# Reordering attention's tail, adding a second set of partial sums in the ELU stage, and loading the output weights in pieces

## The reference

```
kv  = einsum('bhsd,bhse->bhde', k, v)
o   = einsum('bhsd,bhde->bhse', q, kv)
x   = o / sqrt(mean(o*o, -1) + 1e-6) * g_norm      # -> [4608, 512]
x   = (sigmoid(x @ w_gate) * (x @ w_val)) @ w_out  # inner width 1536
h   = x @ w_in                                     # inner width 2048
out = where(h > 0, h, exp(min(h, 0)) - 1) @ w_out2 # [4608, 512]
```

## Time and profile before

| | us |
|---|---|
| median of 3 runs | 1703.28 (1703.05 to 1709.16) |
| profiled execution | 1700.83 |
| its span | 1698.7 |
| TensorE matmul busy | 1639.0 (96%) |
| DVE busy | 1198.8 (71%) |
| ACT busy | 819.1 (48%) |
| GpSimd busy | 181.7 (11%) |

### The profile page before, as it was taken

One profiled execution on the slowest core, in us unless ns is written; L12 is line 12 of the kernel. 1 busy time (PEld: TensorE's weight loads), 2 busy tenths in 40 slices (PEclk: granted clock), 3 DMA queues, 4 the chain that ended last, 5 costly groups with the idle time before them and its releaser, 6 DMA issues.

```text
span 1698.7 us, 27990 instructions
## 1 busy us (share of the span) xinstructions
PE 1639.0 (96%) x10920; PEld 1613.1 (95%) x10920; DVE 1198.8 (71%) x1429; ACT 819.1 (48%) x1251; POOL 181.7 (11%) x185
## 2 busy tenths in 40 slices
PE   6996999999999999999999999999999899999999
PEld 5776999999999999999999999999999799999999
DVE  5777888887588754777777666776765676766764
ACT  6664555554455443444444444554454444444443
POOL 6564222220022100000000000000000000000000
PEclk9998999999999999999999999999999999999999
DMA  9993488878788456554333754423329833333341
GB/s 279 283 293 130 161 309 314 311 292 318 257 302 313 175 180 228 206 226 142 137 137 140 284 193 140 149 105 138 139 103 347 300 128 125 125 124 125 133 145 55
DMA packets 194745, 339.35 MB, mean 200 GB/s; under 512 B 13376, under 2 KB 149568, under 8 KB 194624
## 3 DMA queue, kind: packets, MB, share of 16 engines
q1 hardware_dynamic: 194624, 337.69, 56.6%
HBM read 191.89 MB, written 145.75 MB: 199 GB/s over the span
## 4 chain that ended last, share of the span: by engine, by line
PE 75%; DVE 6%; ACT 4%; issue 4%; DMA 2%; SPq 1%; POOL 0%; ACTq 0%; DVEq 0%; POOLq 0%
PE pair L898 38%; PE pair L963 21%; PE pair L931 15%; DVE s L1393 3%; DVE e L1498 2%; ACT e L1187 1%; DMA u_elu<-s 1%; ACT s L1206 1%; ACT e L1223 1%; ACT e L1218 1%; DMA wreg<-weight_items 1%; DMA weight_items<-out_w 0%; ACT s L1197 0%; ACT ring L1083 0%; SPq L493 0%
## 5 line engine op out<-in xcount | busy, mean ns | idle before, releaser
L898 PE MATMUL pair<-ring,wreg 128*128 128x384 f32 x5040 | 887.7, 337 | 25.5 <-ACT s L1206 15.5
L898 PEld LDWEIGHTS pair<-ring,wreg 128*128 128x128 f32 x5040 | 879.7, 189 | 32.6 <-ACT s L1206 20.9
L963 PE MATMUL pair<-wreg,ring 128*128 128x256 f32 x3024 | 364.8, 284 | 6.6 <-DMA wreg<-weight_items 6.6
L963 PEld LDWEIGHTS pair<-wreg,ring 128*128 128x128 f32 x3024 | 364.6, 193 | 6.8 <-DMA wreg<-weight_items 6.8
L1393 DVE TENSOR_TENSOR s<-s,pair 128x768 f32<-128x768 f32 (+1 forms) x252 | 210.7, 836 | 179.4 <-PE pair L898 144.3
L931 PE MATMUL pair<-ring,wreg 128*128 128x384 f32 x1512 | 262.2, 334 | 0.0
L931 PEld LDWEIGHTS pair<-ring,wreg 128*128 128x128 f32 x1512 | 262.1, 188 | 0.0
L1317 DVE TENSOR_TENSOR ring<-raw,ring 128x1024 fp32r<-128x1024 f32 (+1 forms) x162 | 180.7, 1134 | 112.3 <-ACT ring L1093 97.3
L1187 ACT ACTIVATE e<-e 128x768 f32<-128x768 f32 x72 | 61.0, 847 | 185.9 <-DVE e L1498 185.9
L1093 ACT ACTIVATE ring<-raw 128x1024 fp32r<-128x1024 f32 x108 | 111.8, 1051 | 55.7 <-DVE raw L1351 41.3
L1317 DVE TENSOR_TENSOR ring<-sum,ring 128x768 fp32r<-128x768 f32 (+1 forms) x90 | 92.3, 1038 | 30.2 <-ACT ring L1093 13.5
(11 more groups left out here) (98 smaller groups left out, 1475.5 us busy)
## 6 DMA issues: line engine op xcount, KB each, us to landing
wreg<-weight_items SPq DMA_DIRECT2D x98, 512.0 KB, 6.8
raw<-u_elu SPq DMA_DIRECT2D x36, 1024.0 KB, 7.4
u_gated<-ub SPq DMA_DIRECT2D x144, 192.0 KB, 2.8
u_elu<-s SPq DMA_DIRECT2D x72, 384.0 KB, 2.4
weight_items<-out_w SPq DMA_DIRECT2D x50, 512.0 KB, 4.6
weight_items<-out_x SPq DMA_DIRECT2D x48, 512.0 KB, 4.7
x_raw<-x_attention SPq DMA_DIRECT2D x48, 384.0 KB, 5.2
raw_k<-u_gated SPq DMA_DIRECT2D x6, 2304.0 KB, 8.4
```

The lines of the kernel that those rows point to most:

```text
L898: mm = pe.matmul(dst[:, g, 0:NT], w[:, a, cols], ring[:, slot, b, kt, :], start=(i in STARTS and kt == a == b == 0), stop=(kt == 1 and a = ...
L963: mm = pe.matmul(dst[:, 0, 0:256], s[:, b, 2 * c + kt, :], w[:, a, cols], start=(i in STARTS and c == kt == a == b == 0), stop=(c == 3 and ...
```

## The change

- The small buffers of attention are laid out anew, so that rinv, r_hi and r_lo no longer lie under s1, s5 and s2. ACT copies P1 after step 33 and P6 after step 35, P5 first after attention. TensorE does P6 directly behind P2, and steps 35 and 36 after it.
- S3, S2, S1, S4 of the first superblock stand after steps 25, 26, 27, 28, the splits of P1 and P2 after steps 28 and 29, the others at 32 to 36. SP loads the superblock after step 24 instead of 28. GpSimd makes three of chunk 1's four sums after steps 25, 26 and 27.
- In the ELU stage even units use s1b, s5b, s2b, odd ones s1, s5, s2; copies wait for the store of two units before. P1's split of the next superblock moves from unit j = 3 (i = 0) to j = 2 (i = 6). raw4_1's first half is loaded in unit 65 instead of 64.
- Output weights: in each unit of the last visit SP loads the cells of that unit's own buffer after P2 (two cells), P7 (three) and P4 (two). In unit 65 the last two follow after the unit and after raw4_1's second half.

```diff
-                 ("sq", [P, 2, HN], F32, 69 * KIB),
...
+                 ("rinv", [P, HN], F32, 69 * KIB),
+                 ("r_hi", [P, 2, HN], F32R, 69 * KIB + 1152),
+                 ("r_lo", [P, 2, HN], F32R, 69 * KIB + 3456),
+                 ("sq", [P, 2, HN], F32, 69 * KIB + 5760),
+                 ("sq_hi", [P, 2, 2, HN], F32R, 69 * KIB + 8064),
+                 ("sq_lo", [P, 2, 2, HN], F32R, 69 * KIB + 12672),
...
+                ("s1b", [P, 2, NT], F32, 69 * KIB),
+                ("s5b", [P, 2, NT], F32, 72 * KIB),
+                ("s2b", [P, 2, NT], F32, 75 * KIB),
...
+        def parts3(n):
+            return {"11": s1b, "12": s2b, "22": s5b} if n % 2 == 0 else {"11": s1, "12": s2, "22": s5}
...
@@ SP @@
-                if p == PAIRS - NP:
+                if p == PAIRS - RING:
...
-                    if j > 0 and at == 0 and last:
-                        sp.wait_ge(s_prod, prod(n - 1, P4))
-                    if j == 2 and at == 0 and last:
+                    if n == FIRST4 - 1 and at == 2:
+                        for m in range(4):
+                            sp.wait_ge(s_st[m], 16 * n)
                         load_raw4(1, (0,))
...
-                    if last and j > 0:
-                        load_out_cells(BUF3[j - 1], pieces)
+                    if last and at > 0:
+                        items = ((0, 1), (2, 3, 4), (5, 6))[at - 1]
+                        if n < FIRST4 - 1:
+                            sp.wait_ge(s_prod, prod(n, items[-1]))
+                            load_out_cells(BUF3[j], items)
+                        elif at < 3:
+                            sp.wait_ge(s_prod, prod(n, items[-1]))
+                            load_out_cells(BUF3[j], items)
                     store_elu(n, c)
             sp.wait_ge(s_prod, prod(FIRST4 - 1, P4))
-            load_out_cells(BUF3[3], range(4))
             for c in range(2):
                 sp.wait_ge(s_st[c], 16 * FIRST4)
             load_raw4(1, (1,))
-            load_out_cells(BUF3[3], range(4, 7))
+            load_out_cells(BUF3[3], (5, 6))
@@ GpSimd @@
-            static_steps(step, PAIRS - RING, PAIRS + LM + 1)
-            for c in range(1, CHUNKS):
+            static_steps(step, PAIRS - RING, PAIRS - RING + 2)
+            weight_sums(1, (0,))
...
+            static_steps(step, PAIRS - RING + 4, PAIRS + LM + 1)
+            weight_sums(1, (3,))
+            for c in range(2, CHUNKS):
                 weight_sums(c)
@@ TensorE @@
             gated_product(0, P2)
-            static_steps(step, PAIRS + 3, PAIRS + 4)
             gated_product(0, P6)
-            static_steps(step, PAIRS + 4, PAIRS + 5)
+            static_steps(step, PAIRS + 3, PAIRS + 5)
@@ ACT @@
+            def first_unit():
+
+                copy_p5(0)
+                fill1(0, 0)
+                fill1(0, 1)
+                sigmoid(0, "11")
...
@@ in fill3, ACT and DVE @@
-                elif j == UNITS3 - 1 and vis + 1 < NS:
+                elif j == UNITS3 - 2 and vis + 1 < NS and i == 6:
+                    split_x2(vis + 1, P1)
+                elif j == UNITS3 - 1 and vis + 1 < NS and i > 0:
                     split_x2(vis + 1, i)
@@ elu_unit, ACT; the same for "12" and "22" @@
-                act.wait_ge(s_st[0], 16 * n)
+                act.wait_ge(s_st[0], 16 * (n - 1))
                 if n == FIRST3:
                     act.wait_ge(s_sum, summed(2, NS - 1, "S4"))
-                act.activation(s1[:, :, :], pa[:, :, 0:NT], ACT.Copy).then_inc(s_snap, 1)
+                    act.wait_ge(s_lo, split2(NS - 1, P4, 2))
+                act.activation(part["11"][:, :, :], pa[:, :, 0:NT], ACT.Copy).then_inc(s_snap, 1)
@@ end of attention, ACT @@
+                if p == PAIRS + 1:
+                    act.wait_ge(s_ms, PAIRS)
+                    copy_p1(0)
+                if p == PAIRS + 3:
+                    copy_p6(0)
+                for i in {PAIRS - 4: (P1,), PAIRS - 3: (P2,), PAIRS: (P6,), PAIRS + 1: (P5,), PAIRS + 2: (P7,),
+                          PAIRS + 3: (P3,), PAIRS + 4: (P4,)}.get(p, ()):
                     split_x1(0, i)
-            act.wait_ge(s_ms, PAIRS)
-            act.wait_ge(s_rlo, B)
-            for n in range(FIRST2):
+            first_unit()
+            for n in range(1, FIRST2):
                 gated_unit(n)
@@ DVE @@
+            def first_unit():
+
+                combine(0, "11", s1[:, :, :], PC[:, :, 0:NT])
+                combine(0, "22", s5[:, :, :], PA[0][:, :, 0:NT])
+                fill1(0, 0)
+                fill1(0, 1)
+                gate(0, "11")
...
-                for name in {PAIRS - 2: ("S3", "S2"), PAIRS + 1: ("S1",), PAIRS + 2: ("S4",)}.get(p, ()):
-                    sum_x(1, 0, name)
+                if PAIRS - 7 <= p < PAIRS - 3:
+                    sum_x(1, 0, SUMS[p - (PAIRS - 7)])
```

More of the change, by code:

```diff
@@ L766, in _, with weight_sums @@
             pool.wait_ge(s_const, CONSTANTS)
-            def weight_sums(c):
+            def weight_sums(c, parts=range(4)):
                 t1, t2 = (by_item(staging(c)[1][:, n, :], c) for n in range(2))
                 b11, b12, b21, b22 = (quarter(c, kh, fh) for kh in range(2) for fh in range(2))
[L772 to L778, removed]
-                pool.wait_ge(s_wsum, 4 * c + 3)
-                pool.wait_ge(s_wlo, ITEMS * c + P2 + 1)
-                pool.tensor_tensor(b21, b21, t2, ALU.subtract).then_inc(s_wsum, 1)
+                if 0 in parts:
+                    if c >= 1:
+                        pool.wait_ge(s_wlo, ITEMS * (c - 1) + P5 + 1)
+                    pool.wait_ge(s_wraw[c % 2], raw_loaded(c))
+                    pool.tensor_tensor(t1, b12, b11, ALU.subtract).then_inc(s_wsum, 1)
+                if 1 in parts:
+                    pool.tensor_tensor(b12, b22, b12, ALU.subtract).then_inc(s_wsum, 1)
+                if 2 in parts:
+                    pool.wait_ge(s_wsum, 4 * c + 1)
+                    pool.tensor_tensor(t2, b22, t1, ALU.subtract).then_inc(s_wsum, 1)
+                if 3 in parts:
+                    pool.wait_ge(s_wsum, 4 * c + 3)
+                    pool.wait_ge(s_wlo, ITEMS * c + P2 + 1)
+                    pool.tensor_tensor(b21, b21, t2, ALU.subtract).then_inc(s_wsum, 1)
             def step(trip, r, valid):
@@ L1131, in gated_unit @@
                     act.wait_ge(*c21_taken(n - 1))
-                act.activation(sg[:, :], pa[:, 0, 0:NT], ACT.Sigmoid).then_inc(s_sig, 1)
+                act.activation(sg[:, :], PA[n % 2][:, 0, 0:NT], ACT.Sigmoid).then_inc(s_sig, 1)
+            def first_unit():
[3 more added lines that the diff above has]
+                sigmoid(0, "11")
+                fill1(0, 2)
+                sigmoid(0, "22")
+                fill1(0, 3)
+                fill1(0, 4)
+                sigmoid(0, "12")
+                fill1(0, 5)
+                fill1(0, 6)
+                sigmoid_c21(0)
+            def gated_unit(n):
+                fill1(n, 0)
+                copy_p1(n)
+                fill1(n, 1)
+                sigmoid(n, "11")
+                fill1(n, 2)
+                copy_p6(n)
+                fill1(n, 3)
+                copy_p5(n)
+                fill1(n, 4)
+                sigmoid(n, "22")
+                fill1(n, 5)
+                sigmoid(n, "12")
+                fill1(n, 6)
+                sigmoid_c21(n)
             def mid_unit(n):
@@ L1489, in elu_unit @@
                 e0, e1 = e_3
+                part = parts3(n)
                 def minimum(c, e, acc):
@@ L1505, in elu_unit @@
                 fill3(n, 0)
-                combine(n, "11", s1[:, :, :], PC[:, :, 0:NT])
-                minimum("11", e0, s1)
+                combine(n, "11", part["11"][:, :, :], PC[:, :, 0:NT])
+                minimum("11", e0, part["11"])
                 fill3(n, 1)
-                result(0, e0, s1)
+                result(0, e0, part["11"])
                 fill3(n, 2)
                 fill3(n, 3)
-                combine(n, "22", s5[:, :, :], pa[:, :, 0:NT])
-                minimum("22", e1, s5)
+                combine(n, "22", part["22"][:, :, :], pa[:, :, 0:NT])
+                minimum("22", e1, part["22"])
                 fill3(n, 4)
-                result(1, e1, s5)
-                combine(n, "12", s2[:, :, :], PB[:, :, 0:NT])
-                minimum("12", e0, s2)
+                result(1, e1, part["22"])
+                combine(n, "12", part["12"][:, :, :], PB[:, :, 0:NT])
+                minimum("12", e0, part["12"])
                 fill3(n, 5)
-                result(2, e0, s2)
+                result(2, e0, part["12"])
                 fill3(n, 6)
```

97 lines of the change are left out of this document (51 added, 46 removed).

## The result

The changed kernel takes 1696.39 us in the median of 8 runs (1691.59 to 1697.99), the kernel before 1703.4 (8 runs, 1702.91 to 1709.16). The ratio is 0.9947, 95% interval [0.9937, 0.9957]: so 7 us faster by the medians and 9 by the ratio, where I forecast 25. The direction was right, the size not; 1696.39 lies outside my range of 1667 to 1691. The profiled execution after took 1696.32 us (span 1694.2), the one before 1700.83.

What follows compares the result with a forecast made beforehand. TensorE was taken as the bound nearly everywhere, with time to win only at its gaps or halved clock. 12.8 + 6.3 - 0.8 + 6.8 = 25.1 us off 1703.28 gave about 1678, range 1667 to 1691.

Steps and rivals of the forecast that it cites:

- P1 to P7: Unit 0 at attention's end: replay from P1's start at 139.7 to P7's at 153.2, before the 4.5 us shift.
- The pipeline reaches step 30 4.5 us later.: Attention steps 25 to 29: sums and splits moved there, x_raw's landing and GpSimd delay step 30 by 4.5 us (bounds 1, 8).
- the uneven fit: Attention steps 25 to 29: six moved sums and splits fit DVE's idle time in total but not evenly; 1.5 us charged.
- Unit 1: "take 1.5.": Unit 1, after attention: DVE's backlog makes P4 come out 1 to 2 us late, taken as 1.5 us lost.
- Second set: 6.3 less, 0.8 against it.: ELU stage: removed store waits and about 1 us of clock gain 6.3 us; 0.8 us charged for e1's store.
- rival 4: Last visit, ELU stage: e1's store lands late and holds DVE's minimum; 2.8 us in each of four units, 11; chance 0.04.
- Output weights: 6.8.: Start of the output stage: loading in pieces leaves 1.5 of the 6.61 us gap and removes 1.7 us of half clock.
- attention and gated stage 12.8: Term A, attention's tail and first units: 11.6 + 2.7 - 1.5 = 12.8 us less (bounds 3 and 19).
- ELU 5.5: ELU stage: the second set's 6.3 us less, with 0.8 us against it for e1's store.
- the first: Attention's tail: x_raw late, DVE held by GpSimd, clock halving again; term A only about 5, time 1686; chance 0.20.

Runs made afterwards that it cites:

- elu_only: The kernel before with the second set of partial sums (and P1's earlier split) alone: 1700.92 us, ratio 0.9969.
- pieces_only: The kernel before with the output weights in pieces alone: 1701.71 us, ratio 0.9976.
- pool_sums_late: The changed kernel with x loaded after step 20 and GpSimd's four sums for weight 1 all after attention: 1691.88 us, ratio 0.9922.
- e_store_from_act: The changed kernel with the store of quarter 21 (e1) issued from ScalarE's DMA queue instead of SyncE's: 1690.33 us, ratio 0.9913.
- tail_only: The kernel before with attention's part of the change alone: 1701.07 us, ratio 0.9977.
- the two stores: Two kernels, each the changed one with e1's store moved: to ScalarE's queue (1690.33 us), or ahead of its place's weight cells in SyncE's queue (1688.82 us).
- out_no_stale_wait: The changed kernel, first output unit's copy of P6 no longer waiting for the last ELU store of 12: 1694.8 us, ratio 0.9939.

## Why the prediction was wrong, step by step

*P1 to P7.* Right: 13.5 us forecast, 13.87 measured; the waits of the earlier trace rows are gone.

*"The pipeline reaches step 30 4.5 us later."* Wrong, and the largest miss. The reciprocal of the last batch was to start near 148 and started at 156.61. Of these 8.5 us, 3.1 are there already at the fifth reciprocal (98.62 and 101.74), ahead of the moved work: that is the spread between executions, and the execution of before on which my sum stood happened to be early (elu_only 101.70 and pieces_only 101.43, with the same code up to there). The other 5.3 are the step's: the interval 6-7 grew by 8.0 us and 5-6 by 0.9, while 7-8 gave 3.6. I had 2 us for x_raw (3.63 waited, and loaded earlier it is paid in stores of O), 1.0 for GpSimd's sums (2.06 by pool_sums_late), and 1.5 for the uneven fit. I bounded the landing by 5.6 us, from four loads of one execution; here the longest landed after 8.3 us, and after 7.4 to 10.1 in the four other kernels with the load after 24. The four of the earlier trace rows were issued from 127.54 on, just before the DMA share fell (0.61 from 132 to 136); here it was still 1.07 from 120.0 to 126.7.

*Unit 1: "take 1.5."* Measured 3.7 us of gaps and about 1.7 us of halved clock behind them, 5.4 in all (3.7 in e_store_from_act, where the clock held). The mechanism named was right (VectorE owes more than the products last); GpSimd's stretching of VectorE's operations was not in the count.

*Second set: 6.3 less, 0.8 against it.* The 6.3 stand (elu_only 5.8). The 0.8 was the wrong size: 5.3 us by e_store_from_act. This is rival 4's mechanism at the landings that it named (10.3 us measured, 10.4 assumed); I gave it 0.04 because I asked when it would outweigh everything, not what it would cost at its likely size. The ground I had against it, that before the same queues left no such wait, was weak: before, none and three cells were issued in the 8 us ahead of these stores, not five and seven, and the longest landing was 6.6 us.

*Output weights: 6.8.* Measured 3.4. By themselves the pieces give 6.6 (pieces_only); in the changed kernel the next late thing was a copy waiting for a store of the ELU stage, then the weights again at 3.7 us once it is taken away. "Say what is late next" was not asked there.

Forecast against measured, by the pair of profiled executions: attention and gated stage 12.8 and 0.6, ELU 5.5 and 0.5, output 6.8 and 3.4. The pair understates the first. With the old tail the first mid unit starts at 689.39, 692.03 and 690.52 us (before, elu_only, pieces_only), with the new one at 688.81, 686.65, 682.92, 685.15 and 686.72 (changed, tail_only, the two stores, out_no_stale_wait): 4.6 us earlier in the mean, as tail_only's ratio has it (3.9). With 4.6 the three parts add up to 8.5, and the times say 7 to 9. Of the 12.8, then, 8.2 are missing: the interval 5-8 is 53.7 us in the mean of those five where my sum makes it 49.4 (49.54 less the 4.66 of S3 and S2, plus 4.5), and unit 1 took 5.4 instead of 1.5. Of the rivals the first was nearest in kind (x_raw late by 2.5 us more, GpSimd in the way) and had 1686; the fourth came with it. What would have been needed was both at once.

Open: the time of the attention edits one by one is told by intervals of single profiled executions, not by times; their spread is as large as the effects. The ELU stage of tail_only took 638.0 us against 635.3 for the same code: behind the gap of unit 43 (3.67 us there, 3.22 before) the clock cost more (168 matmuls in 32.15 us against 30.73), and behind one of 1.99 us it fell where it had held behind 1.94 (84 in 16.41 against 14.86); why is open. So 0.5 us for the ELU stage carries a spread of that size too.

## What to carry to other kernels

Work moved into a stretch pays that stretch's prices: landing times are read where the transfer will run, beside the DMA share there, and a store issued behind loads in one queue may land late (10.3 us against 2.3 here) and hold whoever needs its buffer, at e1 as at O. When a wait on one buffer is removed, list the other buffers with the same rule and cost each at its likely landing, since one single buffer left (e1) kept most of the old price. Before a sum of edits is added up, run or reckon them in pairs: here the parts alone gave 3.9, 5.3 and 4.1 us by their ratios, 13.3 in sum, and together 9.0; issuing one store ahead of the cells of its place gave 7.3 more, of which the profile shows 3.2 in the ELU stage.

## What the runs showed of the hardware

A store of 384 KB in one queue landed 2.3 us after its issue with no cell issued in the 8 us ahead, and 10.3 us after it with seven weight cells of 512 KB ahead; from the other engine's queue it still took 7.0 to 8.8 us in the same stretch, so a second queue shortens such a landing and does not free it. The clock fell to 0.66 behind an idle time of 3.09 us in unit 1, and to 0.61 behind the 6.84 us (126.7 to 131.5), while gaps of 2.88 and 2.38 us in the ELU stage left it at 1.00, and one of 1.99 us in tail_only did not (0.69 from 1298 to 1301); why 3.09 us halves it in one place, in some executions only (1.00 in the same place in e_store_from_act), these runs do not tell.
